# Expert tiles of an attention and mixture-of-experts kernel: three of them moved ahead of the last block's routing, and router weights folded or not

## The reference, cut to what matters

```python
def reference(q, k, v, w_phi, w1, w2, w3, w_out, w_gate, ew1, ew2):
    # 8 batches x 8 heads x 576 positions, 64 wide; features by w_phi (64 x 128)
    phi = lambda x: exp of +-(x @ w_phi - max|x @ w_phi|), both signs side by side
    kv = phi(k).T @ v; z = phi(k).sum(over positions)
    x = (phi(q) @ kv) / (phi(q) @ z + 1e-6)          # -> 4608 tokens x 512
    # dense part
    x = ((x @ w1) * (x @ w2)) @ w3 @ w_out           # 512 -> 1024 -> 1024 -> 512
    # routed part: 8 experts, each token goes to one
    logits = x @ w_gate                              # 512 x 8
    idx = argmax(logits)
    gate = softmax(logits)[idx]                      # denominator + 1e-9
    out[t] = gate[t] * (relu(x[t] @ ew1[idx[t]]) @ ew2[idx[t]])   # 512 -> 1024 -> 512
```

## Time and profile before

| | |
|---|---|
| profiled execution | 1581.2 us |
| its span | 1579.4 us |
| PE busy | 1520.7 us, 96% of the span |
| PE weight loads | 1314.5 us, 83% |
| DVE, ACT, POOL busy | 838.8, 629.4, 444.5 us |
| granted clock of PE, mean | 0.986 |
| DMA | 135.98 MB, 86 GB/s |

### The profile page before, as it was taken

The page is one execution under the profiler, slowest core; times in us unless marked ns, Lnnn a source line. Parts: engine busy times, 40 slices in busy tenths (PEclk is TensorE's granted clock), DMA queues, the critical chain, the costliest instruction groups (busy, mean ns, idle before and its releaser), DMA issues. The chain is left out here.

```text
span 1579.4 us, 29928 instructions
## 1 busy us (share of the span) xinstructions
PE 1520.7 (96%) x8481; PEld 1314.5 (83%) x8482; DVE 838.8 (53%) x1616; ACT 629.4 (40%) x1339; POOL 444.5 (28%) x613
## 2 busy tenths in 40 slices
PE   7999999999989999999999999968999999999996
PEld 5889999999978888888888888856888888888885
DVE  5478888888734563745637456352434434332221
ACT  4368787878742121221212212123434433342221
POOL 1256767667720020120201202111122122112121
PEclk9999999999999999999999999989999999999998
DMA  6334443433540012020120201235323443211110
GB/s 238 123 92 111 102 109 102 107 103 98 145 125 6 28 54 80 0 80 27 53 80 0 80 27 53 70 102 188 124 98 118 153 160 122 100 37 40 44 46 23
DMA packets 84409, 135.98 MB, mean 86 GB/s; under 512 B 50016, under 2 KB 50272, under 8 KB 79890
## 3 DMA queue, kind: packets, MB, share of 16 engines
q1 hardware_dynamic: 76674, 115.06, 23.7%
q0 software_dynamic: 7696, 20.43, 3.9%
HBM read 106.62 MB, written 29.89 MB: 86 GB/s over the span
## 5 line engine op out<-in xcount | busy, mean ns | idle before, releaser
L158 PE MATMUL bank<-big,xs 128*128 (+1 forms) x2112 | 506.8, 396 | 14.8 <-DVE big L416 8.2
L158 PEld LDWEIGHTS bank<-big,xs 128*128 128x128 f32 x2112 | 393.2, 189 | 94.2 <-issue 14.4
L158 PE MATMUL bank<-xs,big 128*128 128x512 f32 x1728 | 396.9, 391 | 2.7 <-PEq L504 2.7
L158 PEld LDWEIGHTS bank<-xs,big 128*128 128x128 f32 x1728 | 324.8, 188 | 70.1 <-issue 2.9
L158 PE MATMUL bank<-big 128*128 128x512 f32 (+1 forms) x1632 | 323.9, 347 | 3.6 <-POOL big L579 2.6
L158 PEld LDWEIGHTS bank<-big 128*128 128x128 f32 (+1 forms) x1632 | 255.0, 164 | 38.0 <-POOL big L579 2.8
L1209 DVE TENSOR_TENSOR arena<-arena,bank 128x512 f32<-128x512 f32 x72 | 49.5, 687 | 245.9 <-PE bank L158 245.9
L1145 DVE CUSTOM_DVE_ANT_0 arena<-arena 128x512 f32<-128x512 f32 x256 | 159.5, 689 | 20.8 <-ACT arena L1105 20.8
L1083 ACT COPY arena<-bank 128x512 f32<-128x512 f32 x72 | 42.4, 589 | 306.5 <-PE bank L158 306.5
L1031 POOL TENSOR_TENSOR arena<-arena 128x512 f32<-128x512 f32 x32 | 37.4, 1181 | 440.7 <-DMA arena<-rec_scratch 440.6
L828 PE MATMUL bank<-v,arena 128*128 128x66 f32 (+1 forms) x1152 | 150.4, 272 | 7.1 <-DMA v<-v 3.9
(11 more groups left out here) (150 smaller groups left out, 1338.1 us busy)
## 6 DMA issues: line engine op xcount, KB each, us to landing
arena<-we SPq DMA_DIRECT2D x32, 1024.0 KB, 4.9
kqraw<-kq SPq DMA_DIRECT2D x32, 576.0 KB, 3.7
rows_scratch<-arena SPq DMA_DIRECT2D x36, 256.5 KB
xT_scratch<-arena SPq DMA_DIRECT2D x32, 288.0 KB
v<-v SPq DMA_DIRECT2D x64, 128.0 KB, 2.3
arena<-xT_scratch SPq DMA_DIRECT2D x8, 1024.0 KB, 5.5
arena<-rec_scratch SPq DMA_DIRECT2D x64, 128.0 KB, 3.9
arena<-w3T SPq DMA_DIRECT2D x8, 512.0 KB, 4.3
```

Source lines behind the costliest of these rows:

```text
L158: ins = nc.tensor.matmul(out, left[a], right[b], start=first and n == 0, stop=last and n == 2)
```

## The change

Stage 0 loses the folding of the router weights with its loads, casts and products. SP writes the filler row (the number 4608 in each column) to the last block's places of the row scratch, 4 x 256 KB. The w12 tiles are now taken in their own order.

Stages 2 and 3 become one block. The last block's ids are kept out of the first three tiles of expert 0: before it, DVE adds to expert 0's slots what is missing to 384 (`pad_first`), and where nothing is missing it adds zero. These tiles' rows can be gathered when block 7's ids have landed. The last block's logits come from the rows themselves: PE turns each quarter (`turn_rows`) and multiplies it by w_gate as an f32 product of 8 columns (`router`). PE's new order is at the end of the diff.

```diff
+FIRST = 3
+TMAX = TPE + E - 1 + FIRST
@@ stage 0, SP
-            for h in range(2):
-                sp.dma_start(woutT[...], t["w_outT"]...)
             for u in range(2):
                 sp.dma_start(m["kqraw"][:, u], t["kq"][u]).then_inc(m["kq_in"][u], 16)
-            sp.wait_ge(lists, 32)
+            for q in range(BQ):
+                sp.dma_start(m["rows"][N - BT + q * P:N - BT + (q + 1) * P, :], m["filler"]).then_inc(lists, 16)
+            sp.wait_ge(lists, 32 + 16 * BQ)
@@ stage 0, ACT
                 if j >= 2:
-                    act.wait_ge(g_mm, j - 1)
+                    act.wait_ge(w34_mm, j - 1)
                 act.copy(w3s[:, 0, j % 2], w3st[:, j % 2]).then_inc(w3_hi, 1)
@@ stage 2, SP, behind the turns
+            sp.wait_ge(lg_mm, BQ)
+            load(CPE, 0)
+            sp.wait_ge(ab_lo, FC * NB)
+            load(CPE + 1, 1)
+            sp.wait_ge(rows_out, 16 * BQ * NB)
+            load(CPE + 2, 2)
+            for u in range(2):
+                announce(u, 1)
+            sp.wait_ge(w_lo, CPE)
+            sp.wait_ge(idt_mm, 1)
+            sp.wait_ge(tabs, 1)
+            load(CPE + 3, 3)
...
@@ stage 2, POOL
-            for i in range(NB - 2, NB):
-                scatter_ids(i)
+            scatter_ids(NB - 2)
+            for g in range(FIRST):
+                pool.dma_start(m["ids0f"][:, g:g + 1], m["idtab"][g * P:(g + 1) * P, :]).then_inc(ids0_in, 16)
+            pool.wait_ge(ids0_in, 16 * FIRST)
+            pool.tensor_copy(m["ids0"][:], m["ids0f"][:]).then_inc(ids0_set, 1)
+            pool.wait_ge(ids0_set, 1)
+            pool.wait_ge(rows_out, 16 * BQ * (NB - 1))
+            first_gather(0)
+            for g in range(1, FIRST):
+                pool.wait_ge(gate_set, g)
+                pool.wait_ge(xtr_mm, g)
+                first_gather(g)
+            scatter_ids(NB - 1)
             pool.dma_start(idrows, m["idtab"]...).then_inc(idr_in, 16)
+            pool.wait_ge(y_sb, 2)
+            pool.indirect_dma_start(t["out"], ...ids0[:, 0:1]..., ysb, ...)
             pool.wait_ge(idr_in, 16)
             pool.wait_ge(tabs, 1)
             pool.wait_ge(idt_sb, 1)
             pool.wait_ge(rows_out, 16 * BQ * NB)
-            gather_rows(pool, m, 0)
+            gather(FIRST)
@@ stage 2, ACT, behind the turns
+            relu(0)
+            turned(BQ - 1)
+            rows_high(1)
+            h_high(0)
+            exponents(NB - 1)
+            relu(1)
+            rows_high(2)
+            h_high(1)
+            weights(CPE)
+            relu(2)
+            weights(CPE + 1)
+            h_high(2)
+            rows_high(3)
+            tiles(act, tile)
@@ stage 2, DVE
+            def pad_first():
+                dve.wait_ge(cnt8_mm, 1)
+                dve.tensor_scalar(pad[:, 0:1], x2T_ps[:, 0:1], -1.0, float(FIRST * P), ALU.mult, ALU.add)...
+                dve.tensor_scalar_max(pad[:, 0:1], pad[:, 0:1], 0.0)...
+                dve.tensor_tensor(slots0, slots0, pad[:, 0:1].to_broadcast([P, BQ]), ALU.add)...
...
+            rows_low(1)
+            logits_from_pe()
+            choices(NB - 1)
+            h_low(0, 0)
+            gates_and_slots(NB - 1)
+            h_low(0, 1)
+            rows_low(2)
             ... (first half of the tile table)
+            result(0)
+            for h in range(2):
+                h_low(1, h)
             ... (second half, then the cast of the ids)
+            weights(CPE)
+            result(1)
+            weights(CPE + 1)
+            for h in range(2):
+                h_low(2, h)
+            rows_low(3)
+            result(tiles(dve, tile))
@@ stage 2, PE
-            def router_products(i): ...
-            def turn_logits(i): ...
+            def turn_rows(q):
+                pe.wait_ge(x2_sb, BQ * (NB - 1) + q + 1)
+                ...
+                for c in range(DC):
+                    last = pe.transpose(x2T_ps[:, c * P:(c + 1) * P], x2[:, q, c * P:(c + 1) * P], m["ident"][:])
+            def router(q):
+                pe.wait_ge(x2T_sb, q + 1)
+                for c in range(DC):
+                    last = pe.matmul(lg_ps[:, q * E:(q + 1) * E], x2T[:, q % 2, c], wgate[:, c], ...)
+                    if not more:                     # behind each quarter q of the last block
+                        if q == 0:
+                            pe.wait_ge(ab_f, FC * NB)
+                            x_transpose(0)
+                        if q >= 2:
+                            router(q - 2)
+                        if q >= 1:
+                            turn_rows(q - 1)
...
+            for h in range(2):
+                first_product(0, h, 0, 0)
+            router(2)
+            turn_rows(BQ - 1)
+            x_transpose(1)
+            h_transpose(0)
+            router(3)
+            first_product(1, 0, 0, 0)
+            places(NB - 1)
+            pe.wait_ge(x2T_sb, BQ)
+            pe.matmul(x2T_ps[:, 0:E], m["ones"][:], m["cum"][:, BQ * E:], ...).then_inc(cnt_mm, 1)
+            first_product(1, 1, 0, 0)
+            x_transpose(2)
+            second_product(0, 0, 0)
+            h_transpose(1)
+            for h in range(2):
+                first_product(2, h, 0, 0)
+            second_product(1, 0, 0)
+            pe.wait_ge(slots_done, NB)
+            pe.wait_ge(idr_in, 16)
+            for r in range(3):
+                last = pe.transpose(last_ps[:, r * P:(r + 1) * P], idrows[:, r], m["ident"][:])
+            last.then_inc(idt_mm, 1)
+            h_transpose(2)
+            x_transpose(3)
             last_tile = tiles(pe, tile)
```

More of the change, by code:

```diff
@@ L922, in weights_low, with table @@
                             m["ring"][:, 0, ds(at, CW)].bitcast(F32), ALU.subtract).then_inc(done, 1)
+EX, ROW, CH, T, EARLY = (k * GMAX for k in range(5))
+def table(m, eng, row, g, least, most):
+    return eng.value_load(m["tab"][0:1, ds(g + row, 1)], min_val=least, max_val=most)
 def stage2(nc, m, t):
@@ L971, in stage2, with tiles, chunks, early_chunks @@
         idrows = m["idrows"].rearrange("p (r n) -> p r n", r=3)
+        ring = m["ring"]
+        ahead = m["ahead"]
+        xt, ht = m["xt"].rearrange("p s (c n) -> p s c n", c=DC), m["ht"].rearrange("p s (j n) -> p s j n", j=FC)
+        xg, hs, ysb = m["xg"], m["hs"], m["ysb"]
+        h_ps, xtr_ps, htr_ps, y_ps = m["bank"][0:2], m["bank"][2], m["bank"][3:5], m["bank"][5]
+        HF = FF // 2
+        def tiles(eng, body):
+            n = table(m, eng, T, 0, E - 1 + FIRST, TMAX)
+            with eng.Fori(FIRST, n) as g:
+                body(g)
+            return table(m, eng, T, 1, E - 2 + FIRST, TMAX - 1)
+        def chunks(eng, first, end, body):
+            with eng.If(first < end):
+                with eng.Fori(first, end) as c:
+                    body(c)
+        def early_chunks(eng, g, body):
+            first = table(m, eng, CH, g - 1, CPE, NCH)
+            end = table(m, eng, EARLY, g, CPE, NCH)
+            chunks(eng, first, end, body)
+        def late_chunks(eng, g, body):
+            first = table(m, eng, EARLY, g, CPE, NCH)
+            end = table(m, eng, CH, g, CPE, NCH)
+            chunks(eng, first, end, body)
         def turns(eng, body):
@@ new lines, in scatter @@
+            def scatter(g):
+                row = table(m, pool, ROW, g, 0, E * TPE)
+                pool.tensor_copy(m["ids"][:], m["idall"][:, ds(row, 1)]).then_inc(ids_set, 1)
+                pool.wait_ge(ids_set, g)
+                pool.wait_ge(y_sb, g + 2)
+                pool.sem_inc(turn_taken, 1)
+                pool.indirect_dma_start(t["out"], bass.IndirectOffsetOnAxis(m["ids"][:, 0:1], 0), ysb, None,
+                                        bounds_check=N - 1, oob_is_err=False).then_inc(scattered, 16)
@@ new lines, in written @@
+            def written(count):
+                pool.wait_ge(scattered, 16 * count)
+                pool.sem_inc(y_free, 1)
+            pool.sem_inc(y_free, 1)
+            for g in range(FIRST):
[4 more added lines that the diff above has]
+            pool.wait_ge(rows_out, 16 * BQ * (NB - 1))
@@ L1055, in _ @@
             pool.wait_ge(rows_out, 16 * BQ * NB)
-            gather_rows(pool, m, 0)
+            gather(FIRST)
+            with pool.Fori(1, table(m, pool, T, 2, E - 3 + FIRST, TMAX - 2)) as g:
+                gather(g + FIRST)
+                written(g)
+                scatter(g)
+            before = table(m, pool, T, 2, E - 3 + FIRST, TMAX - 2)
+            last = table(m, pool, T, 1, E - 2 + FIRST, TMAX - 1)
+            written(before)
+            scatter(before)
+            written(last)
+            scatter(last)
+            pool.wait_ge(scattered, 16 * last + 16)
+            pool.wait_ge(gathered, 16 * last + 32)
         @block.scalar
@@ new lines, in relu @@
+            def relu(g):
+                act.wait_ge(gate_set, g + 1)
+                for h in range(2):
+                    act.wait_ge(h_mm, 2 * g + h + 1)
+                    if h == 0 and not (isinstance(g, int) and g == 0):
```

(31 more changed lines are left out.)

510 lines of the change are left out of this document (159 added, 351 removed).

## The result

The changed kernel takes 1587.6 us (median of 20 runs, 1579.1 to 1595.1), the kernel before 1580.8 (20 runs beside them, 1574.0 to 1583.3). The ratio is 1.0047, 95% interval 1.0031 to 1.0063: slower by 0.5%, where I had forecast 1572.3 and faster. The profiled execution took 1591.9 us, 4.3 above its median, and its span is 1590.2.

The account below looks back on a forecast made before the run. PE was taken to be busy nearly all through, so only its work or holes count, at stage 0 and block 8's hand-over. 1581.2 - 2.4 (stage 0) - 6.5 (hand-over) = 1572.3 us, range 1566.5 to 1578.

Parts of the forecast that it names:

- the new waits: Hand-over: gather 0 2.0 us, gather 3 1.0, ids of block 8 0.3, small hand-overs 0.3, taken off 10.1 gained.
- Stage 0: Preparation of the weights: 3.0 us gained without the router folding, 0.6 taken off for filler writes, 2.4 net.
- my bound of 9.6: End of stage 0: slowest landing assumed for the four filler writes, 9.6 us, as in block 7 beside id scatters.
- PE's own work to the lists' transposes: Hand-over, from block 8's first output product: PE's products and transposes in the new order sum to 57.8 us.
- The rival in which they cost double: Block 8's routing: 16 f32 router products cost 0.23 us once more each, 1576.0 us in all; chance 0.05.
- Gather 0: Ahead of tile 0's transpose: PE waits for block 7's ids and the gather, 0 to 5 us, taken as 2.0.
- the "slower" rival: Block 8's output rows: gather 0 comes 15.8 us late and holds up routing, 1586.1 us in all; chance 0.05.
- The ids of block 8: Ahead of the lists' transposes: ids back at 1082.2 against 1083.7, nearly late; 0 to 2.5 us, taken as 0.3.
- Gather 3: Behind the lists' transposes: gather 3 meets three chunk loads, 0 to 1.8 us late, taken as 1.0.
- Behind it: From tile 3's transpose to its first product 2.84 us, then that product at half clock, 7.0.
- small hand-overs: Hand-over: small hand-overs and the added count product together cost 0.3 us.
- the 80.4: Distance from block 8's first output product to the end of tile 3's first product: 80.4 us instead of 86.9.

Follow-up runs that it names:

- the late wait: The changed kernel with stage 0's last SP wait, for the four filler writes, moved to the end of stage 1: 1588.0 us, 1.0054.

## Why the prediction was wrong

The mechanism, one hole in place of several and less work for PE, was right: the kernels that do it without the new waits are 11 to 14.5 us faster than before. The sum of the new waits was wrong. Against the terms of the forecast, in the profiled execution:

- **Stage 0: 2.4 expected, 0.95 came.** The filler writes took 10.6 us (10.1 to 11.4 in nine other traces), past my bound of 9.6, and stage 1 began at 73.6 instead of 72.
- **PE's own work to the lists' transposes: 57.8 expected, 58.8 came** (72.3 less 5.87, 5.33 and 2.32 of half clock). Four blocks of output rows at 5.55 (1045.29 to 1050.84) instead of 5.4 are 0.6 of it. The router products cost what I had said: four f32 products in 0.80 us (1050.84 to 1051.64), eight records, 0.2 each. The rival in which they cost double is refuted, and with it, for this shape, the reading by four passes that I had taken from the Trainium skill, "FP8 and Floating Point Precision", section "TensorE Precision Notes".
- **Gather 0: 2.0 expected, 8.2 came**: 5.87 of hole and 2.32 for a block at half clock behind it. I had 7.9 us for the ids of block 7 (POOL waited 9.37) and 5.3 for the gather (7.7 came, beside the DVE subtraction and the chunk load). Nor had I charged the clock for this hole, though the earlier trace rows show what a hole does to the block behind it. It is the step of the "slower" rival, at a third of its size; in the executions with a hole of 0.6 to 1.4 my 2.0 is right.
- **The ids of block 8: 0.3 expected, 5.3 came.** This is the step that failed most plainly. I took the landing from the earlier trace rows, 7.91 us, where only row writes were beside them and DMA was busy for a quarter of the time. In the changed kernel SP issues two chunk loads of 1 MB between 1073.2 and 1074.4, among the four scatters, and a third at 1081.0: POOL waited 13.0 us, in eight other traces with the loads there 13.6 to 15.8, and in seven without them 7.0 to 8.2. I had charged gather 3 for the loads beside it and not the ids.
- **Gather 3: 1.0 late expected, 0.6 early came**: 9.40 us from the lists' transposes to its own, where I had 9.04 and 1.0.
- **Behind it: 2.84 expected, 8.26 came**, and then 8.26 instead of 7.0 for the product. The forecast said "done with its waits at 1079" of DVE and "no others over 1 us". I had followed the copies of y as far as their time and not as far as their buffer: `result(1)` needs `y_free`, POOL gives it in `written(1)`, this stands behind gather 4, and that one waits for the gate of tile 3. So the copy of tile 1 waits for gather 3. The forecast had put this term at nothing. No view of the kernel before could show it; the order of POOL's and DVE's lines in the changed kernel does.

Together: gather 0 6.2, ids 5.0, own work 0.7 (the 0.3 of small hand-overs taken off), gather 3 -0.6, y buffer 5.4, its product 1.3: 18.0 us over the 80.4, which gives the 98.2 to 0.2; with 1.4 for stage 0 it is 1591.7, where 1591.9 was measured. The median, 1587.6, is 4.3 us lower; what the other executions save is not shown.

Of the four waits, the one for the ids is shown by an edit: with the loads out of the way POOL waits 7 to 8 us instead of 13 to 16, and the ratio falls by 0.0065 in both comparisons (10.6 us in the one with both kernels on one chip). That edit changes DVE's order too, and 3.4 us of its gain are at tile 3's product. The y buffer is shown in the trace (7.14 to 1.95); the ratio falls by 0.0026, about 4.1 us, but the intervals overlap. The 1 to 3 us that stage 0 gains in the traces of the late wait appear in no median, and the intervals are too wide to rule them out; where they go I have not found. The part between stage 0 and the hand-over takes 945.8 to 954.0 us from one execution to the next, which is more than what is looked for. It doesn't go with the start of stage 1: 945.8 follows the latest start, 76.41, and 948.6 the earliest, 69.97.

## What to carry to other kernels

When a step is moved, look up what the other queues issue in its new place: a landing time read where DMA was busy for a quarter of the time was half of what it became beside three loads of 1 MB, and moving the loads, with the splits that belong to them, gave back more than the whole loss in one comparison and three quarters of it in the other. Follow each wait of a moved instruction to the instruction that frees its buffer, and read what stands ahead of that one in its engine's order. Price a hole of PE with the block behind it: behind the holes of 5 us and more the block of 24 took 7.2 to 8.3 us here instead of 5.6.

## What the runs showed of the hardware

- Four id scatters of 128 rows, 4 bytes each, were waited for 7.0 to 8.2 us behind the last of them, and 13 to 15.8 with loads of 1 MB among them. They took 7.3 us even with a DMA share of 0.00 in that time; 2052-byte rows written ahead of them made no difference that can be seen (7.6 us without).
- The indirect gather's instruction on GpSimd took 1.0 to 1.1 us, and 2.8 to 3.1 where a DVE subtraction of 2048 columns from SBUF had begun before it; in all six such executions it ended 0.9 us behind the end of that subtraction. A copy of one column on GpSimd took 1.24 us instead of 0.18 in the same company (at 1099.91 above; it ended within 0.1 us of DVE's subtraction of 1098.81).
- Two kernels each stood 0.3% higher against the kernel before in one comparison than in another (1.0080 and 1.0047; 1.0015 and 0.9982). The intervals overlap, so a difference between the chips is not shown.
